# First unit of the mixture by plain products as heads arrive; one bias per head pair in the lead, token zeros on ScalarE, normalisation in two parts

## What is computed

```
# q, k, v: [4, 8, 576, 64]
scores = q @ k.T / sqrt(64) + slope[h] * -|i - j|   # only 0 <= i - j < 128
attn   = exp(scores - max);  attn /= attn.sum(-1) + 1e-9
x      = (attn @ v), heads side by side             # [2304, 512]

# first mixture: 4 experts, w1 [4, 512, 1024], w2 [4, 1024, 512]
p = domain_probs / (domain_probs.sum(-1) + 1e-9)
out = sum_e p[:, e] * (relu(x @ w1[e]) @ w2[e])

# second mixture, with 32 slots in all: logits = out @ phi, softmax over
# tokens into the slots, 8 small experts, softmax over slots back to tokens
```

## Time and profile before

| | us |
|---|---|
| median of 3 runs | 998.73 |
| lowest, highest | 997.78, 1002.35 |
| the profiled execution, its own time | 997.73 |
| its span in the trace | 995.9 |

### The profile page before, as it was taken

How to read it: one execution, slowest core, us unless ns; L and a number is a source line. 1 busy time by engine, 2 the same in 40 slices (tenths; PEclk the granted TensorE clock), 3 DMA queues, 4 the chain that set the end, 5 groups by cost and what they waited for, 6 DMA issues and landing times.

```text
span 995.9 us, 18516 instructions
## 1 busy us (share of the span) xinstructions
PE 957.9 (96%) x6067; PEld 793.7 (80%) x6067; DVE 596.0 (60%) x1175; ACT 446.6 (45%) x943; POOL 659.6 (66%) x587
## 2 busy tenths in 40 slices
PE   8879999999999989999999999989999999999896
PEld 6558888888888878888888888878888899887532
DVE  5895556565565776556566565665655656556602
ACT  4774444444444544444444444634434344432312
POOL 5988676667669796666667668797866676661000
PEclk8799999999999989999999999999999999999998
DMA  8633314214214213314214212119212122137896
GB/s 251 187 92 114 107 43 128 91 42 130 88 48 126 89 43 112 109 43 127 92 42 130 88 46 82 43 50 333 73 56 84 42 84 69 58 104 283 348 377 238
DMA packets 86403, 116.90 MB, mean 117 GB/s; under 512 B 6208, under 2 KB 56896, under 8 KB 86352
## 3 DMA queue, kind: packets, MB, share of 16 engines
q1 hardware_dynamic: 84736, 109.89, 33.9%
q0 software_dynamic: 1616, 6.36, 1.7%
...
## 4 chain that ended last, share of the span: by engine, by line
PE 82%; POOL 7%; DVE 4%; issue 4%; DMA 1%; ACT 1%; DVEq 0%; SPq 0%; POOLq 0%; ACTq 0%
PE banks L1364 36%; PE banks L1346 32%; PE banks L1304 3%; PE banks L1256 2%; POOL h_lo L665 2%; PE banks L1497 1%; PE banks L1524 1%; PE banks L1278 1%; POOL ws_lo L656 1%; PE banks L1280 1%; DVE w_lo L1043 1%; POOL w_lo L656 1%; PE banks L1237 1%; DMA out<-slot_w 1%; PE banks L1423 1%
## 5 line engine op out<-in xcount | busy, mean ns | idle before, releaser
L1071 DVE SCALAR_TENSOR_TENSOR acc<-banks,prob,acc 128x512 f32<-128x512 f32 x288 | 215.5, 748 | 191.4 <-PE banks L1364 191.2
L1364 PE MATMUL banks<-w_hi,h_hi 128*128 128x512 f32 x576 | 227.1, 394 | 5.0 <-POOL h_lo L665 2.7
L1364 PE MATMUL banks<-w_hi,h_lo 128*128 128x512 f32 x576 | 229.2, 398 | 0.0
L1364 PE MATMUL banks<-w_lo,h_hi 128*128 128x512 f32 x576 | 228.4, 396 | 0.0
L665 POOL TENSOR_TENSOR h_lo<-c,h_hi 128x384 fp32r<-128x384 f32 x144 | 149.8, 1057 | 103.4 <-ACT c L842 103.2
L840 ACT ACTIVATE h_hi<-c 128x384 fp32r<-128x384 f32 x144 | 75.0, 521 | 169.5 <-PE banks L1364 100.6
L656 POOL TENSOR_TENSOR ws_lo<-w_sum,ws_hi 128x1024 fp32r<-128x1024 f32 x48 | 117.0, 2438 | 33.4 <-ACT ws_hi L816 33.4
L1346 PE MATMUL banks<-xT_hi,ws_hi 128*128 128x384 f32 x384 | 131.3, 342 | 3.1 <-POOL ws_lo L656 3.1
L1346 PE MATMUL banks<-xT_lo,ws_hi 128*128 128x384 f32 x384 | 129.1, 336 | 0.0
L1346 PE MATMUL banks<-xT_hi,ws_lo 128*128 128x384 f32 x384 | 128.8, 335 | 0.0
L1364 PEld LDWEIGHTS banks<-w_hi,h_hi 128*128 128x128 f32 x576 | 108.7, 189 | 23.9 <-issue 9.2
...
## 6 DMA issues: line engine op xcount, KB each, us to landing
...
```

The costliest lines, as they stand in the source:

```text
L1071: dve.scalar_tensor_tensor(acc[:, tile, :], ps_y[tt % 2][:, :], prob[:, tile, bass.ds(e, 1)], acc[:, tile, :], ALU.mult, ALU.add).then_inc ...
L1364: ins = pe.matmul(ps_y[tt % 2][:, :], hh[:, f, tt * P:(tt + 1) * P], wp[u % 2][:, f, :], start=m == 0, stop=m == 3 * FT - 1)
```

## The change

- **Unit 0 by plain products.** The up part of unit 0 in pass 0 is four plain products (two hidden halves by two token halves; `plain`, `PLAIN`), each over four head pairs, 3 matmuls a pair: 48 matmuls of 384 columns where there were 42. They read x itself, not the sums. `plain(0)` and `plain(1)` over three head pairs stand at v = 24 and 25 (9 matmuls each; before it was 3 each), and after the lead 3 + 3 + 12 + 12 remain (before: 36). Each has a PSUM bank, and relu and the split come from the bank; no `add_product`, no `u1`.
- **x is split by head pair.** ACT rounds a whole pair (768 columns, `x_head_hi`) at v = 7, 13, 19, 23, DVE subtracts (`x_head_rest`) at v = 8, 14, 20, 23. The sums T1 to T4 are first needed by unit 1. POOL makes them for kk = 0 at v = 14 and for kk = 1 after the lead (before: DVE, at v = 23). T1 has a place of its own in `xt`. ACT and DVE split them after the lead, 768 columns at once, between the relus of unit 0.
- **Weights.** Unit 0 needs no sums of w1: `w1_sums(0)` and the second part of its split fall away. Those of unit 1 move into the lead (v = 15 to 20) from behind it.
- **One bias per pair in the lead**: pairs alternate between the two buffers. The body keeps two per pair.
- **Zeros by ScalarE**: six copies of 512 columns at scale 0 where POOL had one memset of 3072 columns, in pass 0 between the relus, later at t = 44, 46, 47, 48, 50, 51. DVE waits for all six before the pass's body.
- **`norm` in two parts**: per head a multiplication by a per-partition scalar, in place of one multiplication of both heads by a broadcast tensor. In the body too.
- **Idle transposes**: 8 at the start in place of 46, and 4, 12, 8, 8, 6, 4 behind the scores of steps 0 to 5 (`FILL`).
- w2's preparation and that of w1 move by one to two turns.

The diff, cut to what is spoken of:

```diff
-            xt = sb("xt", [P, 3, 2, TB])
+            xt = sb("xt", [P, 4, 2, TB])
...
+        FILL = {0: 4, 1: 12, 2: 8, 3: 8, 4: 6, 5: 4}
...
         def bias_at(v):
-            if (v + 8) % ATT == 0:
-                n, late = (v + 8) // ATT, 0
-            elif (v + 4) % ATT == 0:
-                n, late = (v + 4) // ATT, 1
...
+            n = (v + 9) // ATT
+            return n if (v + 9) % ATT == 0 and 0 < n <= KD + 1 else None
...
-        ZERO_AT = 45
+        ZERO_AT = [44, 46, 47, 48, 50, 51]
...
+        PLAIN = [(0, 0), (1, 0), (0, 1), (1, 1)]
+        ps_plain = [bank[6], bank[7], bank[2], bank[1]]
+        T_ORDER = [1, 3, 4, 5]
...
         def _(pool):
...
             def norm(p, n, a, lead):
                 pool.wait_ge(s_rinv, place(n, a) + 1)
-                pool.tensor_tensor(buf[:, :, 0:w], buf[:, :, 0:w],
-                                   rinv[:, a, :].unsqueeze(2).broadcast_to([P, 2, w]),
-                                   ALU.mult).then_inc(s_norm, 1)
...
+                for h in range(2):
+                    ins = pool.tensor_scalar(buf[:, h, 0:w], buf[:, h, 0:w], rinv[:, a, h:h + 1], None,
+                                             ALU.mult)
+                ins.then_inc(s_norm, 1)
...
-                if v == 6:
-                    w1_sums(0, 0, 0)
-                if v == 9:
+                if v == 8:
                     w1_rest(0, 0, 0, 0)
-                if v == 11:
-                    w1_rest(0, 0, 0, 1)
-                if v == 13:
+                if v == 14:
                     pool.wait_ge(s_oc, FROM + 4)
                     combine_x(0, slice(0, 1), 0)
-                if v in (16, 18, 20):
-                    x_rest(0, 0, v // 2 * 2 - 15, slice(0, 1))
-                if v == 21:
+                if v == 16:
                     w1_sums(0, 0, 1)
-            for n in (1, 3, 5):
-                x_rest(0, 1, n, slice(1, 2))
-            w1_rest(0, 0, 1, 0)
-            w1_rest(0, 0, 1, 1)
-            zero(0)
+                if v == 18:
+                    w1_rest(0, 0, 1, 0)
+                if v == 20:
+                    w1_rest(0, 0, 1, 1)
+            pool.wait_ge(s_oc, FROM + 2 * KD)
+            combine_x(0, slice(1, 2), 4)
...
         def _(act):
+            def zero(p, tt):
...
+                act.activation(acc[:, p * NTP + tt, :], ident[:, 0:1].broadcast_to([P, D]), ACT.Copy,
+                               scale=0.0).then_inc(s_zero, 1)
...
+                if v in (7, 13, 19):
+                    x_head_hi(HEADS[v // 6 - 1])
...
+                if v == STEPS - 1:
+                    x_head_hi(HEADS[KD - 1])
+            plain_hi(0)
+            plain_hi(1)
+            t_hi(1)
+            plain_hi(2)
+            for tt in range(TT):
+                zero(0, tt)
+            plain_hi(3)
+            for tt in range(TT, NTP):
+                zero(0, tt)
+            for n in T_ORDER[1:]:
+                t_hi(n)
             for p in range(PASSES):
...
         def _(dve):
-                if v == 13:
+                if v == 11:
                     w2_rest(0, 0, 0)
-                if v in (15, 17, 19, 21):
-                    x_rest(0, 0, v - 15, slice(0, 1))
...
+                if v in (8, 14, 20):
+                    x_head_rest(HEADS[v // 6 - 1])
+                if v == STEPS - 1:
+                    x_head_rest(HEADS[KD - 1])
+            plain_rest(0)
+            plain_rest(1)
...
+            x_rest(0, 1)
+            plain_rest(2)
...
+            plain_rest(3)
+            for n in T_ORDER[1:]:
+                x_rest(0, n)
             for p in range(PASSES):
-                dve.wait_ge(s_zero, p + 1)
+                dve.wait_ge(s_zero, NTP * (p + 1))
...
         def _(pe):
-            keep_warm(46, bank[1])
+            keep_warm(8, bank[5])
...
+                if j in FILL:
+                    keep_warm(FILL[j], bank[5])
                 if v in (LEAD - 3, LEAD - 2):
                     pe.wait_ge(s_neg, FROM + LEAD)
-                    product(0, 0, 0, v - LEAD + 3, (0,))
+                    pe.wait_ge(s_w1lo, 2)
+                    plain(v - LEAD + 3, HEADS[:-1])
...
-            for n in range(NPROD):
-                product(0, 0, 0, n, (1,) if n < 2 else (0, 1))
+            for i in range(4):
+                plain(i, HEADS[-1:] if i < 2 else HEADS)
```

236 lines of the change are left out of this document (132 added, 104 removed).

## The result

The changed kernel is **slower by 0.4%**: a median of 1002.5 us (20 runs) against 998.5 us (20 runs), ratio 1.004 [1.0031, 1.005]. The forecast was 991.0, with 985 to 996.5 as its range: wrong in sign, and out of the range. The profiled execution of the changed kernel took 1006.0 us (span 1004.2). I read from the traces where the time goes, and from the medians how much it is. Where a part of the changed kernel is longer than forecast, some of it can belong to that one execution.

What follows compares the result with a forecast made beforehand. TensorE bounds the body almost without waits; time was to be won in the lead, in its waits and half clock. Gains of 6.1 + 0.8 + 0.8 = 7.7 us off 997.73 gave 990.0, a median of 991.0, range 985 to 996.5.

Steps and rivals of the forecast that it cites:

- I take 0.70: POOL's norm in the lead: two 192-column parts take 0.70 us together, against 0.845 for the old one; upper end 1.2.
- Rival 2: Norm at the two-input price, POOL bounding from the sums on: 3 us lost, 994; chance 0.30 shared with two other rivals.
- POOL rows of 0.6 us: Sign of a wrong forecast: POOL's norm rows at 0.6 us each, where 0.35 was expected.
- Part D: Attend 16 to the lead's end: 20.4 us before, 19.4 forecast, with 1.8 us of waits left; gain 1.0, bounds -1.5 and 2.8.
- Part B: Attend 4 to scores 16: 11.75 us before and the same after, k arriving as late; gain 0, bounds -1 and 0.6.
- Part C: Scores 16 to attend 16: 15.1 us before, 12.0 forecast, half of 6.2 us of waits and half clock going; gain 3.1.
- Rival 1: Clock stays low or drops again from scores 16 to attend 16: 3 to 5 us lost, 994 to 996; shared chance 0.30.
- Part A: Start to attend 4: 24.84 us before, 22.8 forecast; gain 2.0, bounds 5 and -5.
- rival 3: Idle transposes don't hold the clock, the lead runs at half: slower, 1011 if it lasts ten steps; chance 0.06.
- rivals 1, 2 and 5: Together 0.30, all at 993 to 997; the fifth: plain form does not come off, 2.3 us lost behind the lead, 994.
- Behind the lead: Lead's end to unit 1's third product: 11.6 us before, 10.8 forecast; gain 0.8, bounds -1.5 and 1.5.
- Ends of passes: At two pass ends, shorter norms and T1 no longer waiting for T3: 0.4 us each, 0.8 in all, bounds 0 and 3.

Runs made afterwards that it cites:

- e1: Changed kernel with the old normalisation, one multiplication of both heads by a broadcast tensor: 997.6 us, ratio 0.9996 to the kernel before.
- e13: e11 with the change's two-part norm put back: 992.1 us, ratio 0.9945 to the kernel before.
- e2: Kernel before with only the two-part normalisation added: 1008.9 us, ratio 1.0123.
- e4: Changed kernel plus 36 small POOL operations of several forms at its very end; row times count (757 ns by scalars, 192 columns), its total says nothing.
- e3: Changed kernel with each half of the norm a two-input multiplication by a broadcast column: 999.5 us, ratio 1.0012 to the kernel before.
- e5: Changed kernel with old norm, POOL's two low parts of unit 1's weights moved behind its last norm: 0.5% or 5 us under e1.
- e6: Changed kernel with old norm, the probabilities' normalisation moved from v = 12 to v = 24: 0.2% or 2 us under e1, not separated by the intervals.
- e7: Changed kernel with old norm, the edits of e5 and e6, and the pair's own q and k (b half) loaded before the next head: 0.7% under e1.
- e8: Changed kernel with old norm and old start (46 idle transposes ahead, none between scores): attend 4 at 21.7 us; no total given.
- e14: e11 with the old start of 46 idle transposes ahead, none between scores: 987.5 us, ratio 0.9903 to the kernel before.
- e12: Kernel before with the probabilities' normalisation behind the lead and q and k (b half) loaded before the next head: lead ends at 69.6 us; no total given.
- e15: Kernel before with POOL's first bias of pair 1 moved from behind the first norm to behind the third: 999.4 us, ratio 1.0023.
- e11: e7 with first four token sums behind POOL's last norm and first-pass zeros by one POOL memset: lowest median, 1.1% under the kernel before.

## Why the prediction was wrong, step by step

**The price of a `norm`: the term that set the sign.** The step was "I take 0.70", with 1.2 as its upper end; it measured 1.50. Rival 2 had the mechanism and 3 us for it; the runs give 4.4 (e1), 5.5 (e13) and 12 (e2). What failed is the choice of the nearest row. I priced a multiplication by the one-input row I had, a select of 402 ns for 256 columns, and took the two-input price for the worst case. e4 shows that one-input forms on POOL are far from alike, 337 ns for a copy and 757 for this multiplication of the same 192 columns. The count of inputs was no bound at all; the 1.2 us for the two-input form would have held (e3 has 2 x 0.52), but the form used is dearer still. The prediction had named "POOL rows of 0.6 us" as a sign of being wrong, and they are 0.78.

**Part D without the norm.** 19.4 us were forecast, and with the old norm the order of the change takes 24.5 (e1). TensorE's own work was right, 17.6 us forecast and 17.5 busy in e5. That e5 also takes 19.4 in all is in part luck: its waits are 1.6 us for ACT and 0.7 for POOL where 1.8 for POOL were forecast, and the two low parts (4.7 us), which the forecast counted in, are moved behind the last `norm` there. The failed step is "It stays close to what PE needs, so 1.8 remain": I compared totals over the part, and the change puts its two low parts of weights ahead of the last `norm`s, not behind them. A queue's total says when it ends, and TensorE waits for what stands in the middle. That the low parts hold up DVE's `rsum` as well (2.25 us for 0.23) was not in the sum either. The waits then came in pieces of 1 to 2 us with half clock beside them (a mean of 0.86 over 24.4 us, so 3.4 us of a full clock's work), which the step did not count.

**Part B.** "Whatever is quicker here, k comes as late after attend 4" was said of scores 16. The changed kernel has no wait there; e6 and e3 have one, and it ends 11.6 and 12.0 us after their attend 4. The load that now counts is the one of scores 10, and nothing in the diff makes that load start earlier. It is issued at 18.8 us and lands 6.6 us later; before it was 18.2 and 5.6, so that it was there at 23.8, and was used at 25.47 without waiting (timeline of before):

```profile
25.47 0.38 PE L1256 MATMUL banks<-k_b,q_b 64*64 64x192 f32 x2
```

After the change it is used at 25.38, behind a wait of 2.38. The 2.5 us by which attend 4 came earlier were gone 3 us later, and half clock (a mean of 0.57 from 25.3 to 33.2) made it 3.8. e1, with the same loads, has the k 5.7 us after 17.9, a wait of 1.1, no half clock behind it, and a B of 11.5, as forecast. So the overlooked load costs 1 to 2.4 us, and whether the rest comes of the two-part `norm` or of this one execution stays open. In e7, with the load put ahead, no wait for k is left. I had asked what is late next only at the wait that the trace of before showed.

**Part C.** 12.0 forecast, 14.1 measured, 14.4 in e1. Rival 1 came true: half clock from 43.5 to 50 us, as in the earlier trace rows. The probabilities' multiplication fell as said, from 2.03 us to 0.43, but behind DVE's low part of w2 the row of five still ends too late. With them apart (e6) C takes 11.8.

**Part A.** 22.8 forecast, 22.3 measured, at a granted clock of 1.00, so rival 3 fell. But that it is 2.5 us under before is in the main luck. The start's transposes win nothing (e8 and e14 have attend 4 at 21.7 with the old start). Nor is it mainly a bias: of the reasons given only the full clock carries the gain, and the change isn't needed for it. The trace of before ran at half clock from 14.0 to 20.8, and e12, with TensorE's and POOL's order of before up to there and no half clock, has attend 4 at 22.08, as early as the changed kernel. What a bias is worth is some 0.8 us, and there it is pair 1's first, behind the first `norm` (e15), not the second of pair 0.

**Behind the lead** 10.1 against 10.8 forecast, with a wait for `u` of 0.6 us where 1 to 1.5 was named. **Ends of passes**: 0.8 forecast; from the third product on the traces have 911.8 after, 912.2 before and 912.9 in e1, but also 911.7 in e11 and 914.8 in e7, whose body is the same, so that 0.8 us can't be told here. TensorE's wait for POOL's low part is there as before:

```profile
PE banks L1423 <- POOL ws_lo L681: 2.0, 1, 2.0
```

**The sum.** 7.7 us forecast. The miss is 7.7 + 4.0 = 11.7. The norm is 4.4 of it. The rest by e1's trace against the forecast: D 5.1 and C 2.4 too long, A 1.0, B 0.3 and the piece behind the lead 0.7 shorter, 912.9 for 911.4 from there on: 7.0. D and C are in the main waits that moved, and I had given rivals 1, 2 and 5 together 0.30 as if they were alternatives. They are not: the first two make each other likelier, since a late POOL makes TensorE wait and the clock falls beside its waits.
